# Experts' x tiles from the fifth on, transposed by a transfer of two-byte planes

## The chip, the core and the metric

One core of one Trainium2 chip runs the kernel. The metric is the device time of one execution in microseconds (us); lower is better.

## The reference

Three stages follow one another; all data are float32.

```python
x = _attn_ref(q, k, v, mem_k, mem_v)     # windowed attention, 4 x 8 x 768 x 64, as rows: 3072 x 512
x = _moe_ref(x, w_in, w_out, a, b)       # h = x @ w_in (2048); rational function of h; @ w_out (512)
# last stage, 8 experts of 1024:
logits = x @ w_gate
expert_idx = argmax(logits, 1)
for e in range(8):
    xe = x[expert_idx == e]
    out[expert_idx == e] = gate_w[:, None] * (maximum(xe @ w1[e], 0) @ w2[e])
```

## The kernel before, in words

Every float32 product is made in three parts: an operand is split into an upper part (rounded by ScalarE) and a lower part (the rest, by VectorE), and upper x upper, upper x lower and lower x upper are summed in PSUM. The stages before the experts end at about 670 us. They leave the rows of x sorted by expert in DRAM (`rows_by_expert`, 514 columns: 512 of x, the gate weight and the row's number), in tiles of 128 rows. The run has 27 tiles of 5 experts, the largest expert first.

The expert stage runs one loop on each engine (`Fori(2, ...)`), which share counters only through semaphores; each engine's work is in the order in which it is written. Tiles 0 to 3 are written out ahead of the loop. Body t of TensorE's loop (lines 816 to 829) is: `transpose_h(t)`, 8 transposes of the hidden layer into PSUM; `first_product(t + 1)`, 24 matmuls with 512 columns, x of the next tile by w1; `transpose_x(t + 2)` (line 535), 4 transposes of the gathered rows into PSUM; `second_product(t)`, 24 matmuls, h by w2.

ScalarE in body t (1035 to 1042): `upper_h(t)`, the upper part of the transposed h; where the schedule says so, `split_expert`, upper parts of 8 chunks of the next expert's weights (128x1024 each; `x_raw` is chunk 0, `e_raw` the seven others); `relu(t + 1)`; `upper_x(t + 2)` in two halves. VectorE (1411 to 1417): `lower_h(t)`, the lower parts of the same 8 chunks, `lower_x(t + 2)`, and `finish(t)`, which multiplies y by the gate weight. `first_product(t + 2)` of the next body waits for `xg_lo_done`, that is for `lower_x(t + 2)`, half by half. The weights' reloads are issued by SyncE as chunks come free (line 507).

POOL (1565 to 1570) in body t: `fetch(t + 3)`, which keeps two columns of the rows before, waits until TensorE has transposed them (`tx_done`) and issues the load of the next 128 rows into `xg`; `land_y(t - 1)` waits for the last store; `copy_idx(t)`; `send_y(t)` waits for `finish(t)` and issues the scatter of y.

Of the kernel before, what the change touches and what calls it, by code (L numbers as in the profile page):

```python
# [15 lines left out]
F32, F32R, BF16, I32, U32 = (mybir.dt.float32, mybir.dt.float32r, mybir.dt.bfloat16,  # L16
                             mybir.dt.int32, mybir.dt.uint32)
ALU = mybir.AluOpType
# [6 lines left out]
P = 128  # L25
# [166 lines left out]
def build(nc, qk_all, v_all, w_mlp, w_exp, w_gate, coef, consts, sights, out):  # L192
# [4 lines left out]
    with ExitStack() as ctx:  # L197
# [80 lines left out]
        with ExitStack() as ph:  # L278
            xg_hi = sb("xg_hi", [P, KT, P], F32R, ph)
            xg_lo = sb("xg_lo", [P, KT, P], F32R, ph)  # L280
# [15 lines left out]
        with ExitStack() as ph:  # L296
            sb("below_ge", [P, 2 * KT * P + (WCH - 1) * CW + 3 * EF + DM], F32, ph)
            ge = sb("ge", [P, 3, TMAX, E], F32, ph)
# [44 lines left out]
        meta_copied, gathered, tx_done = (sem(n) for n in ("meta_copied", "gathered", "tx_done"))  # L343
        xg_hi_done, xg_lo_done, w1e_done = sem("xg_hi_done"), sem("xg_lo_done"), sem("w1e_done")
# [166 lines left out]
        def _(pe):  # L511
# [304 lines left out]
            with pe.Fori(2, before_last) as t:  # L816
# [6 lines left out]
                transpose_x(t + 2)  # L823
# [11 lines left out]
            pe.sem_inc(tx_done, 2)  # L835
# [20 lines left out]
        def _(act):  # L856
# [68 lines left out]
            def upper_x(t):  # L925
# [4 lines left out]
                for c in range(2):  # L930
                    act.wait_ge(tx_done, t * 2 + (c + 1))
                    act.activation(xg_hi[:, 2 * c:2 * c + 2].rearrange("p k t -> p (k t)"),  # L932
                                   PS[:, x_halves(t)[c], 2 * c * P:2 * (c + 1) * P], ACT.Copy).then_inc(xg_hi_done, 1)

# [100 lines left out]
            with act.Fori(2, last_tile) as t:  # L1035
                act.wait_ge(w2e_done, upto(w2e_done, t))
                upper_h(t)
                nxt = load_sched(act, R_SPLIT, t, 0, E - 1)
# [3 lines left out]
                upper_x(t + 2)  # L1042
# [5 lines left out]
        def _(dve):  # L1048
# [108 lines left out]
            def lower_x(t):  # L1157
# [5 lines left out]
                for c in range(2):  # L1163
                    dve.wait_ge(xg_hi_done, t * 2 + (c + 1))
                    dve.tensor_tensor(xg_lo[:, 2 * c:2 * c + 2].rearrange("p k t -> p (k t)"),  # L1165
                                      PS[:, x_halves(t)[c], 2 * c * P:2 * (c + 1) * P],
                                      xg_hi[:, 2 * c:2 * c + 2].rearrange("p k t -> p (k t)").bitcast(F32),
# [243 lines left out]
            with dve.Fori(2, last_tile) as t:  # L1411
# [4 lines left out]
                lower_x(t + 2)  # L1416
# [6 lines left out]
        def _(pool):  # L1423
# [30 lines left out]
            def keep_meta(t):  # L1454

                pool.wait_ge(gathered, t * 16 + 16)
                pool.tensor_copy(meta_of(t, slice(0, 2)), xg[:, DM:XW]).then_inc(meta_copied, 1)

# [102 lines left out]
            tiles = load_sched(pool, R_CNT, 0, NSUB, TILES)  # L1561
            fetch(4, col)
            send_y(1)
            fetched, before_last, last_tile = tiles_less(pool, 3), tiles_less(pool, 2), tiles_less(pool, 1)
            with pool.Fori(2, fetched) as t:
                fetch(t + 3, col_of(t + 3))
                land_y(t - 1)
                copy_idx(t)
                pool.drain()
# [3 lines left out]
            pool.wait_ge(gathered, tiles * 16)  # L1573
            pool.tensor_copy(meta_of(last_tile, slice(0, 2)), xg[:, DM:XW]).then_inc(meta_copied, 1)
# [86 lines left out]
```

## Time and profile before

| | us |
|---|---|
| median of 3 runs | 997.41 (997.26 to 997.83) |
| profiled execution, own time | 995.93 |
| its span, first to last instruction | 993.9 |
| TensorE busy | 976.4 (98%) |
| VectorE busy | 619.0 (62%) |
| ScalarE busy | 580.9 (58%) |
| POOL busy | 403.9 (41%) |
| mean granted TensorE clock | 0.999 of full |

The times of rows below count from the span's start. PE is TensorE's matmuls and PEld its weight loads, DVE is VectorE, ACT ScalarE, SP SyncE; a q behind the name (ACTq) is the engine's instruction queue, where issues of transfers and scalar operations are. L541 is line 541. Busy time of an engine says nothing by itself of what waits for what; the chain of waits does: it goes back from the last instruction, at each step to what released it.

### The profile page before, as it was taken

To read this page: it belongs to the slowest core of one execution; us is meant where nothing else is said; L and a number is where in the kernel's file an instruction comes from. 1 tells how busy PE (TensorE), PEld (TensorE's weight loads), DVE (VectorE), ACT (ScalarE), POOL (GpSimd) and SP (SyncE) were. 2 spreads that over 40 slices of the span, in tenths; PEclk is the share of its full clock that TensorE was granted. 3 is DMA by queue.
4 is the path that set the end of the run, shared out by engine and by line. 5 is a ranking of instruction groups with operands and counts; after the bars stand their busy time and mean duration, and the time that the engine had idled before them with its cause. 6 is when DMAs were issued, how large, how long until landed. Compare 5 with 4: busy or idle time off the path is not lost. (4 is left out here: it accounts for less than half of the span.)

```text
span 993.9 us, 19287 instructions
## 1 busy us (share of the span) xinstructions
PE 976.4 (98%) x6102; PEld 797.9 (80%) x6103; DVE 619.0 (62%) x1073; ACT 580.9 (58%) x1248; POOL 403.9 (41%) x393
## 2 busy tenths in 40 slices
PE   7999999999999999999999999999999999999997
PEld 5787778888887888888888888887888888888886
DVE  6786788767876876697678778862524324325222
ACT  6998787766676676676676767831524224225221
POOL 2886454444654464446446544732111111111111
PEclk9999999999999999999999999999999999999999
DMA  8999415920990194059001301215812412411100
GB/s 288 392 398 402 175 43 180 367 91 1 306 362 10 59 369 166 0 173 335 0 0 42 116 24 40 67 43 165 281 47 78 176 42 75 169 42 42 33 32 26
DMA packets 58031, 140.49 MB, mean 141 GB/s; under 512 B 4663, under 2 KB 10423, under 8 KB 57984
## 3 DMA queue, kind: packets, MB, share of 16 engines
q1 hardware_dynamic: 51120, 119.06, 33.8%
q0 software_dynamic: 6560, 20.77, 6.2%
q8 instruction: 28, 0.46, 0.2%
q14 instruction: 19, 0.16, 0.0%
q10 hardware_dynamic: 304, 0.04, 0.0%
HBM read 68.32 MB, written 72.32 MB: 142 GB/s over the span
## 5 line engine op out<-in xcount | busy, mean ns | idle before, releaser
L524 PE MATMUL PS<-xs,weights 128*128 (+1 forms) x1152 | 280.8, 392 | 0.0
L524 PEld LDWEIGHTS PS<-xs,weights 128*128 128x128 f32 x1152 | 213.6, 188 | 44.0
L686 PE MATMUL PS<-weights,g_hi 128*128 128x512 f32 x768 | 237.9, 391 | 0.9 <-POOL g_lo L1497 0.3
L1497 POOL TENSOR_TENSOR g_lo<-g_sb,g_hi 128x512 fp32r<-128x512 f32 x96 | 125.1, 1303 | 263.7 <-ACT g_hi L993 263.7
L686 PEld LDWEIGHTS PS<-weights,g_hi 128*128 128x128 f32 x768 | 143.0, 188 | 34.3 <-POOL g_lo L1497 2.8
L686 PE MATMUL PS<-weights,g_lo 128*128 128x512 f32 x384 | 149.5, 389 | 0.0
L974 ACT ACTIVATE b_ln<-PS,cf 128x512 f32<-128x512 f32 x96 | 66.0, 687 | 131.2 <-PE PS L524 131.2
L567 PE MATMUL PS<-weights,h_hi 128*128 (+1 forms) x432 | 136.2, 396 | 1.4 <-DVE h_lo L1174 1.4
L558 PE MATMUL PS<-weights,xg_hi 128*128 (+1 forms) x432 | 136.2, 396 | 0.8 <-issue 0.5
L1500 POOL TENSOR_TENSOR den<-den,b_r 128x512 f32<-128x512 f32 x96 | 128.1, 1334 | 3.9 <-ACT b_r L1001 3.6
L1210 DVE SCALAR_TENSOR_TENSOR den<-den,b_r 128x512 f32<-128x512 f32 x96 | 66.0, 687 | 76.6 <-POOL den L1500 76.5
L567 PEld LDWEIGHTS PS<-weights,h_hi 128*128 128x128 f32 x432 | 79.0, 188 | 17.4 <-issue 1.4
L558 PEld LDWEIGHTS PS<-weights,xg_hi 128*128 128x128 f32 x432 | 79.0, 188 | 17.0 <-issue 1.2
L1165 DVE TENSOR_TENSOR xg_lo<-PS,xg_hi 128x256 fp32r<-128x256 f32 x52 | 19.6, 418 | 116.5 <-ACT xg_hi L932 116.5
L944 ACT ACTIVATE h_sb<-PS 128x1024 f32<-128x1024 f32 x27 | 27.6, 1023 | 110.2 <-PE PS L558 110.2
L939 ACT ACTIVATE h_hi<-PS 128x512 fp32r<-128x512 f32 x54 | 29.3, 596 | 104.3 <-PE PS L551 104.3
L1531 POOL DMA_INDIRECT out<-y_sb,idx_s x27 | 27.5, 1018 | 149.3 <-DVE y_sb L1186 146.3
L558 PE MATMUL PS<-weights,xg_lo 128*128 (+1 forms) x216 | 84.6, 392 | 0.0
L567 PE MATMUL PS<-weights,h_lo 128*128 (+1 forms) x216 | 84.5, 391 | 0.0
L686 PEld LDWEIGHTS PS<-weights,g_lo 128*128 128x128 f32 x384 | 72.1, 188 | 15.2
L980 ACT ACTIVATE num<-PS,neg_a 128x512 f32<-128x512 f32 x96 | 74.9, 780 | 0.0
L1246 DVE SCALAR_TENSOR_TENSOR den<-b_ln,b_r 128x512 f32<-128x512 f32 x96 | 66.0, 688 | 13.8 <-ACT b_r L977 11.6
(209 smaller groups left out, 1511.2 us busy)
## 6 DMA issues: line engine op xcount, KB each, us to landing
rows_by_expert<-pad_rows SPq DMA_DIRECT2D x16, 1799.0 KB
e_raw<-w_exp SPq DMA_DIRECT2D x34, 512.0 KB, 6.5
qk<-qk_all SPq DMA_DIRECT2D x32, 420.0 KB, 6.1
rows_by_expert<-pad_rows SPq DMA_DIRECT2D x8, 1542.0 KB
vw<-v_all SPq DMA_DIRECT2D x32, 384.0 KB, 6.2
rows_by_expert<-pad_rows SPq DMA_DIRECT2D x8, 1285.0 KB
w_raw<-w_mlp SPq DMA_DIRECT2D x16, 512.0 KB, 7.6
pad_rows<-rows_by_expert POOLq DMA_DIRECT2D x27, 257.0 KB
```

Of the source, the lines that this page charges most:

```text
L524: last = pe.matmul(PS[:, H_BANK + f % 2, :], w[:, wp], rhs, start=k == 0, stop=k == 3 * KT - 1)
L558: last = pe.matmul(PS[:, half, :], xp[:, kt, :], w_half(off, kt, wp, half), start=n == 0, stop=n == 3 * KT - 1, skip_group_check=True)
L567: last = pe.matmul(PS[:, y_bank(t), :], hp[:, ft, :], w_half(off, KT + ft // 2, wp, ft % 2), start=ft == 0 and k == 0, stop=ft == EKT - 1 ...
L686: last = pe.matmul(PS[:, ACC_BANK + s, :], gp[:, f % 2, s * P:(s + 1) * P], w[:, wp], start=f == 0 and k == 0, stop=f == FT - 1 and k == 2)
L939: act.activation(hi[:, 4 * c:4 * c + 4].rearrange("p k t -> p (k t)"), PS[:, h_banks(t)[c], :], ACT.Copy).then_inc(h_hi_done, 1)
L944: act.activation(h_sb[:], PS[:, 0:2, :].rearrange("p a n -> p (a n)"), ACT.Relu).then_inc(relu_done, 1)
L974: act.activation(b1_ln[:], PS[:, hb, :], ACT.Abs, scale=cf[:, 4:5]).then_inc(b12_done, 1)
L980: act.activation(num[:, par], PS[:, hb, :], ACT.Identity, scale=neg_a[:, 3:4], bias=neg_a[:, 2:3]).then_inc(u_done, 1)
L1210: dve.scalar_tensor_tensor(den[:, q], den[:, q], -2.0, b2_r0[:, q], ALU.add, ALU.mult).then_inc(w_done, 1)
L1246: dve.scalar_tensor_tensor(den[:, par], b1_ln[:], 1.0 + 1e-6, b2_r0[:, par], ALU.add, ALU.add).then_inc(q_ready, 1)
L1497: pool.tensor_tensor(g_lo[:, q], g_sb[:], g_hi[:, q].bitcast(F32), ALU.subtract).then_inc(g_lo_done, 1)
L1500: pool.tensor_tensor(den[:, st.m % 2], den[:, st.m % 2], b2_r0[:, st.m % 2], ALU.mult).then_inc(t_ready, 1)
```

## The change

For tiles 4 and up TensorE no longer transposes x. POOL parts the gathered rows (each float32 is two 16-bit halves) into two planes, all lower halves and all upper halves (`planes`, 1,024 two-byte elements a partition; `part_x`). ScalarE's queue issues one transfer that transposes the 8 blocks of 128 x 128 two-byte elements from `planes` to `mirrored` within SBUF (`turn_x`), behind `upper_h` and ahead of `split_expert`. VectorE joins the halves again to float32 in `xt`, in two copies, behind its splits (`join_x`); then `upper_turned` and `lower_turned` make `xg_hi` and `xg_lo` from `xt` in SBUF, as `upper_x` and `lower_x` did from PSUM. `xt` lies where `xg_lo` lies, so the join also waits until the product of the tile before is over (`w1e_done`). The load of the next rows waits for POOL's own parting (`load_next`) in place of TensorE's transposes. ScalarE's and VectorE's loops run one turn past the last tile, so POOL raises `planes_done` once more.

```diff
@@ -277,6 +277,8 @@
             count = sb("count", [P, E], F32, ph)
         with ExitStack() as ph:
             xg_hi = sb("xg_hi", [P, KT, P], F32R, ph)
+            with ExitStack() as over:
+                xt = sb("xt", [P, KT, P], F32, over)
             xg_lo = sb("xg_lo", [P, KT, P], F32R, ph)
             e_raw = sb("e_raw", [P, WCH - 1, CW], F32, ph)
             h_hi = sb("h_hi", [P, EKT, P], F32R, ph)
@@ -295,6 +297,9 @@
             h1_lo = sb("h1_lo", [P, EKT, P], F32R, ph)
         with ExitStack() as ph:
             sb("below_ge", [P, 2 * KT * P + (WCH - 1) * CW + 3 * EF + DM], F32, ph)
+            with ExitStack() as over:
+                planes = sb("planes", [P, 2 * DM], U16, over)
+                mirrored = sb("mirrored", [P, 2 * KT, P], U16, over)
             ge = sb("ge", [P, 3, TMAX, E], F32, ph)
             gt = sb("gt", [P, E, SLOTS], F32, ph)
             per = sb("per", [P, 8, E], F32, ph)
@@ -341,6 +346,7 @@
         e_hi_done, e_lo_done = sem("e_hi_done"), sem("e_lo_done", WCH)
         led.append((e_lo_done, WCH))
         meta_copied, gathered, tx_done = (sem(n) for n in ("meta_copied", "gathered", "tx_done"))
+        planes_done, planes_turned, xt_done, turn_go = (sem(n) for n in ("planes_done", "planes_turned", "xt_done", "turn_go"))
         xg_hi_done, xg_lo_done, w1e_done = sem("xg_hi_done"), sem("xg_lo_done"), sem("w1e_done")
         relu_done, th_done, h_hi_done, h_lo_done = sem("relu_done"), sem("th_done"), sem("h_hi_done"), sem("h_lo_done", 1)
         w2e_done, gate_copied, y_done = sem("w2e_done", 1), sem("gate_copied"), sem("y_done", 1)
@@ -820,7 +826,6 @@
                 transpose_h(t)
                 first_product(t + 1)
                 order, off = load_sched(pe, R_ORD, t, 1, E), load_sched(pe, R_OFF, t, 0, WCH)
-                transpose_x(t + 2)
 
                 pe.wait_ge(h_lo_done, upto(h_lo_done, t * 2 + 2))
                 pe.wait_ge(y_done, upto(y_done, t))
@@ -832,7 +837,6 @@
             pe.wait_ge(h_lo_done, upto(h_lo_done, t * 2))
             transpose_h(t)
             first_product(last_tile)
-            pe.sem_inc(tx_done, 2)
             order, off = load_sched(pe, R_ORD, t, 1, E), load_sched(pe, R_OFF, t, 0, WCH)
             pe.wait_ge(h_lo_done, upto(h_lo_done, t * 2 + 2))
             pe.wait_ge(y_done, upto(y_done, t))
@@ -931,6 +935,18 @@
                     act.wait_ge(tx_done, t * 2 + (c + 1))
                     act.activation(xg_hi[:, 2 * c:2 * c + 2].rearrange("p k t -> p (k t)"),
                                    PS[:, x_halves(t)[c], 2 * c * P:2 * (c + 1) * P], ACT.Copy).then_inc(xg_hi_done, 1)
+
+            def turn_x(t):
+
+                act.wait_ge(planes_done, t - (FIRST_TILES - 1))
+                act.sem_inc(turn_go, 1)
+                act.dma_start(mirrored[:], planes[:], transpose=True).then_inc(planes_turned, 16)
+
+            def upper_turned(t):
+                for c in range(2):
+                    act.wait_ge(xt_done, (t - FIRST_TILES) * 2 + (c + 1))
+                    act.activation(xg_hi[:, 2 * c:2 * c + 2].rearrange("p k t -> p (k t)"),
+                                   xt[:, 2 * c:2 * c + 2].rearrange("p k t -> p (k t)"), ACT.Copy).then_inc(xg_hi_done, 1)
 
             def upper_h(t):
                 hi = h_tiles(t)[0]
@@ -1035,11 +1051,12 @@
             with act.Fori(2, last_tile) as t:
                 act.wait_ge(w2e_done, upto(w2e_done, t))
                 upper_h(t)
+                turn_x(t + 2)
                 nxt = load_sched(act, R_SPLIT, t, 0, E - 1)
                 with act.If(nxt > 0):
                     split_expert(nxt)
                 relu(t + 1)
-                upper_x(t + 2)
+                upper_turned(t + 2)
             act.wait_ge(w2e_done, upto(w2e_done, last_tile))
             upper_h(last_tile)
 
@@ -1167,6 +1184,22 @@
                                       xg_hi[:, 2 * c:2 * c + 2].rearrange("p k t -> p (k t)").bitcast(F32),
                                       ALU.subtract).then_inc(xg_lo_done, 1)
 
+            def join_x(t):
+
+                dve.wait_ge(planes_turned, (t - (FIRST_TILES - 1)) * 16)
+                dve.wait_ge(w1e_done, t)
+                for c in range(2):
+                    dve.tensor_copy(xt[:, 2 * c:2 * c + 2].bitcast(U16).rearrange("p k (t w) -> p k t w", w=2),
+                                    mirrored[:].rearrange("p (w k) t -> p k t w", w=2)[:, 2 * c:2 * c + 2]).then_inc(xt_done, 1)
+
+            def lower_turned(t):
+                for c in range(2):
+                    dve.wait_ge(xg_hi_done, t * 2 + (c + 1))
+                    dve.tensor_tensor(xg_lo[:, 2 * c:2 * c + 2].rearrange("p k t -> p (k t)"),
+                                      xt[:, 2 * c:2 * c + 2].rearrange("p k t -> p (k t)"),
+                                      xg_hi[:, 2 * c:2 * c + 2].rearrange("p k t -> p (k t)").bitcast(F32),
+                                      ALU.subtract).then_inc(xg_lo_done, 1)
+
             def lower_h(t):
                 hi, lo = h_tiles(t)
                 for c in range(2):
@@ -1413,7 +1446,8 @@
                 nxt = load_sched(dve, R_SPLIT, t, 0, E - 1)
                 with dve.If(nxt > 0):
                     split_expert(nxt)
-                lower_x(t + 2)
+                join_x(t + 2)
+                lower_turned(t + 2)
                 finish(t)
             lower_h(last_tile)
             finish(last_tile, last_y)
@@ -1455,6 +1489,20 @@
 
                 pool.wait_ge(gathered, t * 16 + 16)
                 pool.tensor_copy(meta_of(t, slice(0, 2)), xg[:, DM:XW]).then_inc(meta_copied, 1)
+
+            def part_x(t):
+
+                keep_meta(t)
+                if not isinstance(t, int):
+                    pool.wait_ge(planes_turned, (t - FIRST_TILES) * 16)
+                    pool.sem_inc(rows_go, 1)
+                pool.tensor_copy(planes[:].rearrange("p (w n) -> p n w", w=2),
+                                 xg[:, 0:DM].bitcast(U16).rearrange("p (n w) -> p n w", w=2)).then_inc(planes_done, 1)
+
+            def load_next(t, col):
+
+                pool.wait_ge(planes_done, t - FIRST_TILES)
+                pool.dma_start(xg[:, 0:XW], tiles_dram[bass.ds(col, 1)].rearrange("o p n -> (o p) n")).then_inc(gathered, 16)
 
             def load_tile(t, col):
 
@@ -1558,20 +1606,20 @@
             copy_idx(1)
             pool.wait_ge(sched_ready, 1)
             col = col_of(4)
-            tiles = load_sched(pool, R_CNT, 0, NSUB, TILES)
             fetch(4, col)
+            part_x(4)
             send_y(1)
             fetched, before_last, last_tile = tiles_less(pool, 3), tiles_less(pool, 2), tiles_less(pool, 1)
             with pool.Fori(2, fetched) as t:
-                fetch(t + 3, col_of(t + 3))
+                load_next(t + 3, col_of(t + 3))
                 land_y(t - 1)
                 copy_idx(t)
+                part_x(t + 3)
                 pool.drain()
                 send_y(t)
             land_y(fetched - 1)
             finish_y(fetched)
-            pool.wait_ge(gathered, tiles * 16)
-            pool.tensor_copy(meta_of(last_tile, slice(0, 2)), xg[:, DM:XW]).then_inc(meta_copied, 1)
+            pool.sem_inc(planes_done, 1)
             finish_y(before_last)
             finish_y(last_tile, True)
```

## Rows read from the trace of the kernel before

**Rows 1.** The page, parts 1 and 2: TensorE's busy time and share; granted clock by slice.

```profile
PE 976.4 (98%) x6102; PEld 797.9 (80%) x6103; DVE 619.0 (62%) x1073; ACT 580.9 (58%) x1248; POOL 403.9 (41%) x393
...
PEclk9999999999999999999999999999999999999999
```

**Rows 2.** Chain of waits, an ordinary expert body: start us, length us, engine, output, line.

```profile
853.62 5.49 PE PS L567 x24
859.12 0.87 PE PS L551 x8
...
865.48 0.44 PE PS L541 x4
```

**Rows 3.** Groups of instructions, 690 to 990: busy us, mean ns, idle before.

```profile
L1291 DVE TENSOR_TENSOR weights<-e_raw,weights 128x1024 f32 x28 | 32.1, 1217 | 0.0
```

**Rows 4.** Timeline, a body with splits: start us, us, engine, line, operation [idle before].

```profile
761.05 1.09 ACT L939 ACTIVATE h_hi<-PS 128x512 fp32r<-128x512 f32 x2 [4.79 <-PE PS L551]
...
763.84 1.23 DVE L1291 TENSOR_TENSOR weights<-x_raw,weights 128x1024 f32 x1 [0.87 <-ACT weights L923]
764.98 8.03 DVE L1291 TENSOR_TENSOR weights<-e_raw,weights 128x1024 f32 x7
772.93 0.74 DVE L1165 TENSOR_TENSOR xg_lo<-PS,xg_hi 128x256 fp32r<-128x256 f32 x2
...
768.63 1.02 POOL L1520 CAST idx_s<-meta 128x1 uint32 x1
```

**Rows 5.** Chain of waits, the same body.

```profile
760.57 0.87 PE PS L551 x8
...
773.74 2.39 PE PS L558 x10
```

**Rows 6.** Chain of waits, end of the first body with splits.

```profile
711.73 0.30 issue
```

**Rows 7.** Timeline, an ordinary body, VectorE and POOL.

```profile
854.56 0.76 DVE L1165 TENSOR_TENSOR xg_lo<-PS,xg_hi 128x256 fp32r<-128x256 f32 x2 [4.94 <-ACT xg_hi L932]
...
854.88 0.20 POOL L1520 CAST idx_s<-meta 128x1 uint32 x1
860.77 1.02 POOL L1531 DMA_INDIRECT out<-y_sb,idx_s  x1 [5.69 <-DVE y_sb L1186]
```

**Rows 8.** Single lines that issue transfers: duration of the issue ns min/median/max, starts.

```profile
L859 ACTq DMA_DIRECT2D sight<-sights x2: 261/419/577, 0.9 to 1.5; - x2
...
L507 SPq DMA_DIRECT2D e_raw<-w_exp x21: 332/333/756, 706.6 to 847.0; - x21
...
L476 SPq DMA_DIRECT2D rows_by_expert<-pad_rows x32: 507/3514/8428, 160.0 to 450.7; - x32
```

**Rows 9.** Landing: weights (line 507); stores of y (the view of DMA issues).

```profile
DMA to landing us min/median/max: 3.3/6.7/10.9
...
out<-y_sb,idx_s POOLq DMA_INDIRECT x27, 2.8
```

**Rows 10.** Lines with a one-source VectorE operation; groups by form.

```profile
L1056 DVE CAST mask<-sight x2: 441/443/445, 4.6 to 5.2; 4x576 bf16<-4x576 f32 x2
...
L1204 DVE COPY x<-PS 128x512 f32<-128x512 f32 x10 | 6.4, 682 | 0.1
```

**Rows 11.** Groups by form, POOL.

```profile
L1446 POOL CAST weights<-w_raw 128x1024 fp32r<-128x1024 f32 x5 | 5.2, 1038 | 0.0
```

**Rows 12.** Timeline, POOL ahead of the expert loop.

```profile
684.92 0.59 POOL L1464 DMA_DIRECT2D pad_rows<-rows_by_expert  x1 [3.17 <-PE PS L541]
687.94 1.03 POOL L1531 DMA_INDIRECT out<-y_sb,idx_s  x1 [2.43 <-issue]
```

**Rows 13.** Line 1154, the first expert's splits: duration ns min/median/max.

```profile
L1154 DVE TENSOR_TENSOR weights<-e_raw,weights x6: 1217/1394/2312, 603.7 to 653.1; 128x1024 fp32r<-128x1024 f32 x6
```

**Rows 14.** Window of an ordinary body: busy us by engine, clock, DMA share, GB/s.

```profile
852.00:864.00 12.00, 12.00 (x61) 9.98 (x60) 2.85 (x6) 2.67 (x5) 1.98 (x4) 1.00 0.26 96
```

**Rows 15.** Waits of TensorE from 690 on: us in total, times, longest us.

```profile
PE PS L567 <- DVE h_lo L1174: 1.2, 1, 1.2
```

More of the change, by code:

```diff
@@ L14 @@
 import concourse.mybir as mybir
-F32, F32R, BF16, I32, U32 = (mybir.dt.float32, mybir.dt.float32r, mybir.dt.bfloat16,
-                             mybir.dt.int32, mybir.dt.uint32)
+F32, F32R, BF16, I32, U32, U16 = (mybir.dt.float32, mybir.dt.float32r, mybir.dt.bfloat16,
+                                  mybir.dt.int32, mybir.dt.uint32, mybir.dt.uint16)
 ALU = mybir.AluOpType
```

## Prediction

> **What bounds the kernel now.** The page first: TensorE is busy in 98% of the span and its granted clock is at full speed in all 40 slices [rows 1], so what counts is what TensorE does and when it is kept waiting. The chain of waits over an ordinary expert body is TensorE alone [rows 2]: transpose h (0.87 us), first product (24 matmuls of the same kind as the second, 5.49), transpose x (0.44), second product (5.49), together 12.29 us. There are 23 such bodies (t = 2 to 24), and each holds one transpose of x, so the removed instructions lie on the path: 4 x about 0.11 us issued, 0.44 us, and no engine covers them.
>
> Four of the 23 bodies also split an expert's weights (28 splits from e_raw in the loop, seven to a body [rows 3], and one each from x_raw ahead of them). Read one on each engine [rows 4], with T the start of its transposes of h, 760.57 [rows 5]: ScalarE ends upper_h at T+1.6 and goes on to the splits; VectorE waits 0.87 us for the first, starts at 763.84, works without a gap and ends at 773.01 (T+12.4); then it makes xg_lo, the first half done at 773.34. TensorE begins the product that needs it at 773.74 [rows 5]. So the spare time of VectorE in such a body is about 0.4 us, some 0.3 after the hand-off; in the first of the four there is none, TensorE idles 0.30 there [rows 6]. Ordinary bodies have 5 us of idle time ahead of xg_lo [rows 7].
>
> **Removed.** 23 x 0.44 = 10.1 us of TensorE if nothing is late next. In the 19 ordinary bodies I take it whole: 19 x 0.44 = 8.4 us. In the four others TensorE would only arrive 0.44 us earlier at a product whose operand isn't there.
>
> **Added, in an ordinary body.** ScalarE issues the transfer behind upper_h, T+1.6. Its price there, d, is not shown by any transposing transfer. Rows around it: this engine's own small loads took 0.26 to 0.58 us to issue, SyncE's of 512 KB 0.33, and the clearing transfers, 896 runs or more each, 0.51 to 8.4 us with a median of 3.5 (their queue full) [rows 8]. The new one moves 256 KB as 8 blocks for 128 partitions, at least 1,024 runs. The row nearest in runs is the clearing one; between its minimum and its median I take d = 2.0, with ends 0.4 and 3.5. The Trainium skill ("DMA: Bandwidth & Descriptors", in "Why a DMA increments its semaphore by 16 and not by 1") speaks against the change here: a transposing transfer within SBUF costs the older sequencers 262,144 cycles for 8,192 tiles, 32 a tile, beside 512 for a plain transfer and 631 for a small transposing one. The trace shows 0.33 us for a plain one, so 0.65 ns a cycle; were a tile 16 rows by 128 elements, as that page's "DMA Transpose (X-bar)" suggests, there would be 64 tiles, 631 + 2,048 cycles, an estimate of 1.7 us, and the sum would be 2 us to the slow side. No row here shows a transposing one.
>
> From the end of the issue to landing I take 3 us (the store of y lands in 2.8 at the median, 512 KB of weights in 6.7, at most 10.9 [rows 9]). So the planes are there at T+6.6. VectorE may join them from T+6.4 on (first product over, w1e_done). Two joins of 512 two-byte elements: a cast of 576 elements within SBUF took 443 ns, a copy of 512 from PSUM 682 [rows 10]; ends 0.8 and 1.4 together, I take J = 0.83 (SBUF to SBUF, as the first row). With upper_turned beside the second join and half of lower_turned (0.4) behind, xg_lo's first half is done 1.4 us after the join starts, T+8; the product needs it at T+11.85+0.87 = T+12.7. The transfer has room to T+11.3, that is X = 9.7 us from issue to landing. relu on ScalarE comes at T+6.4 and is not behind an issue of 2 to 3.5 us. So an ordinary body pays nothing.
>
> POOL: load_next no longer waits for TensorE's transposes, it is issued behind the store of y, at T+2.7 [rows 7], and the rows land about T+6.4 (3 us as the store, and its own 0.6); part_x waits for the transfer before (T+6.6); 1,024 two-byte elements cost 1.04 us at the rate of its cast [rows 11], 2.1 if two-byte writes go at half of it. Behind it waits send_y, whose y comes only at T+12.7; idle time ahead of it was 5.7 us [rows 7]. Hidden. In front of the loop part_x(4) stands before send_y(1): the rows asked for at 684.92 are there at 688 and parted at 689.5, so y of tile 1 leaves about 2 us later than at 687.94 [rows 12]; its next user is finish(2), at the end of the second product of t = 2 (711.73 less 0.87 and a body of 12.29: 698.6 [rows 2, 6]). Tile 4's planes are turned near 694.5, needed joined at about 699. Hidden, with 2 us left. The 24th turn, of a tile that doesn't exist, is released by POOL about T+4.5 of the last body and joined ahead of finish, which isn't due before T+11.85: nothing.
>
> **Added, in a splitting body.** All of it is in VectorE's full queue. (1) ScalarE's first split starts d later; VectorE already waits for that split, so its whole chain ends d later: 2.0. (2) The joins stand behind the splits and ahead of xg_lo: 0.83. (3) part_x meets the splits: an earlier split of the same size took 1.39 us at the median and 2.31 at most beside POOL's work, 1.22 at least, and POOL's cast of one column took 1.02 instead of 0.20 among the splits [rows 4, 7, 13]. Ends 0 and 1.1, I take 0.3, since POOL's copy is about as long as one split. Less the spare 0.3: 2.83 us added per body (the 0.44 gained is already used up in arriving early), three times, and 3.13 in the first: 11.6. What follows (finish, lower_h) has over 3 us until its product.
>
> **Sum.** -8.4 + 11.6 = +3.2 us. The profiled execution's span of 993.9 becomes 997.1, its own time 995.93 becomes 999.1. The median of the runs lies 1.5 us above that execution; on it I forecast 1000.6 us. Less than 0.2%, 2 us, can't be told from no change.
>
> **Rivals.**
> Cheap issue (other side): the ACT queue issues the transfer as fast as its others, d = 0.44. Its place is the four splitting bodies; each then costs 0.83 + 0.44 + 0.3 - 0.3 = 1.3, 5.4 with the first, against 8.4 gained: 994.4. It decides from d under 0.7 (then over 2 us are gained). For: the only rows of ACT's queue. Against: they move 128 runs or fewer. Chance 0.29. Between d = 0.7 and 1.7 the two sums cancel within 2 us: 0.17, time about 997.
>
> The transfer itself lands too late: above X = 9.7 every body stalls by the excess, since the join stands between landing and product. At the longest landing of the rows, 10.9 [rows 9], each ordinary body pays 1.2 - 0.44: 19 x 0.76 = 14.4, and with the 11.6 of the splitting bodies, whose joins come later than any landing, it is 1023. Against: that landing had seven transfers of 512 KB in flight; DMA engines are 26% busy in an ordinary stretch [rows 14]. Chance 0.10. The Trainium skill ("VectorE: DVE Perf Modes", "The three transpose paths") gives 1309 ns for 128x128 two-byte elements by DMA against 390 on TensorE, and advises TensorE where PSUM will do. Eight blocks one after another would be an estimate of 10.5 us, which is this rival at about 1016.
>
> TensorE's clock: the stalls of some 3.3 us (2.83 + 0.44) are longer than any idle time of the expert stretch; 1.2 us of it left the granted clock where it was [rows 1, 15]. If it fell to the lower level (1.2 of 2.4 GHz) for one product, 5.49 would be 11, four times: +22, 1023. Chance 0.03. The Trainium skill ("TensorE: Matmul & The Clock Gate", "Why this matters for your kernels") warns of gaps between bursts for this reason; no run here shows such a fall.
>
> The forecast itself, d of 1.7 to 3.5: 0.41. That the transposes stay on TensorE is excluded: only tiles up to 3 keep them.
>
> **Range.** Best of the bounds: d 0.44, J 0.8, no contention: 8.4 - 4 x 0.94 - 0.3 = 4.3 gained, 993.1. Worst without rivals: 3.5 + 1.4 + 1.1 - 0.3 = 5.7 per body, 23.1 less 8.4, 1012. I take 992.5 to 1018, half way into the late transfer. Faster 0.29, same 0.17, slower 0.41 + 0.10 + 0.03 = 0.54.
>
> **What would show it.** (a) Ordinary bodies of 11.85 us without a gap in TensorE: right; a wait for xg_lo there: the transfer is late. (b) ScalarE's issue behind upper_h: 2 us, and the first split of the four bodies later by it. (c) Joins of 0.4 us each. (d) TensorE idle about 3.3 us ahead of the product after each splitting body. Under 1.7 us of it, the kernel is faster and my d is wrong. (e) The same clock throughout. (f) part_x of 1 to 2.6 us, and y never late for TensorE.

## The result, and the profile after

The changed kernel takes 1030.91 us (median of 3 runs, 1029.08 to 1030.97) against 997.41: ratio 1.0327, 95% interval 1.0302 to 1.0352. It is slower by 33 us where 3 were forecast, outside the range. The profiled execution took 1029.08 us, span 1027.2.

The page, parts 1 and 2 (compare [rows 1]):

```profile
PE 977.3 (95%) x6010; PEld 796.6 (78%) x6011; DVE 720.1 (70%) x1121; ACT 584.0 (57%) x1248; POOL 521.4 (51%) x416
...
PEclk9999999999999999999999999998998999898999
```

TensorE has some 90 instructions fewer and is busy 0.9 us longer, and four slices late in the span no longer show full speed. VectorE is busy 101 us more, POOL 118. The groups of instructions by form, 690 to 1000, say where:

```profile
L1499 POOL COPY planes<-pad_rows 128x1024 uint16<-128x1024 uint16 x23 | 116.2, 5053 | 0.1
L1198 DVE TENSOR_TENSOR xg_lo<-xt,xg_hi 128x256 fp32r<-128x256 f32 x46 | 64.6, 1440 | 9.3 <-ACT xg_hi L948 8.7
L1324 DVE TENSOR_TENSOR weights<-e_raw,weights 128x1024 f32 x28 | 44.2, 1646 | 0.0
L1192 DVE COPY xt<-mirrored 128x512 uint16<-128x512 uint16 x46 | 41.8, 951 | 88.5 <-PE PS L564 76.5 <-DMA mirrored<-planes 12.0
```

POOL's parting takes 5 us each time, and three kinds of VectorE work have grown in the mean: the splits from 1,217 ns [rows 3] to 1,646, beside xg_lo and the joins. A mean hides the shape of it. Line 1324 in one splitting body, then line 1499 over the whole span (duration min/median/max), and the timeline of that body:

```profile
L1324 DVE TENSOR_TENSOR weights<-e_raw,weights x7: 1209/1210/5244, 779.7 to 790.6; 128x1024 f32 x7
```

```profile
L1499 POOL COPY planes<-pad_rows x23: 4692/4880/5887, 689.6 to 986.4; 128x1024 uint16<-128x1024 uint16 x23
```

```profile
769.12 4.85 POOL L1499 COPY planes<-pad_rows 128x1024 uint16<-128x1024 uint16 x1
...
769.34 4.61 DVE L1198 TENSOR_TENSOR xg_lo<-xt,xg_hi 128x256 fp32r<-128x256 f32 x2 [0.60 <-ACT xg_hi L948]
...
774.45 1.27 ACTq L943 DMA_TRANSPOSE mirrored<-planes  x1
...
778.56 1.22 DVE L1324 TENSOR_TENSOR weights<-x_raw,weights 128x1024 f32 x1 [2.52 <-ACT weights L927]
...
779.71 12.05 DVE L1324 TENSOR_TENSOR weights<-e_raw,weights 128x1024 f32 x7
...
780.92 5.88 POOL L1499 COPY planes<-pad_rows 128x1024 uint16<-128x1024 uint16 x1
...
791.69 0.75 DVE L1192 COPY xt<-mirrored 128x512 uint16<-128x512 uint16 x2
...
792.58 0.76 DVE L1198 TENSOR_TENSOR xg_lo<-xt,xg_hi 128x256 fp32r<-128x256 f32 x2
...
793.25 1.21 PE L564 MATMUL PS<-weights,xg_hi 128*128 x2 [6.27 <-DVE xg_lo L1198]
```

Six of the seven splits take the old 1.21 us and one takes 5.24: it isn't slowed down, it is held, by 4.03, beside the parting of 780.92 to 786.80. Two halves of xg_lo, 0.84 us of work, are held for 4.61 in the ordinary body ahead (769.34) and end with the parting of 769.12, at 773.97. In an ordinary body that costs nothing, there were 4.94 us of idle time [rows 7]. In a splitting one everything is behind it, and TensorE stands for 6.27 us.

What TensorE does after that, in windows (busy us and count of PE, PEld, DVE, ACT, POOL, then granted clock, DMA share, GB/s):

```profile
788.00:793.00 5.00, 0.00 (x0) 0.00 (x0) 4.85 (x8) 0.87 (x3) 0.00 (x0) 0.75 0.88 258
793.00:797.00 4.00, 3.75 (x9) 2.98 (x10) 2.36 (x6) 0.97 (x2) 1.11 (x2) 0.50 0.98 361
797.00:801.00 4.00, 4.00 (x19) 3.26 (x18) 0.07 (x1) 0.07 (x1) 1.66 (x4) 0.95 0.59 169
```

The granted clock is 0.50 (1.2 GHz) for the first 4 us of the product, which does 9 matmuls there instead of 19. The chain of waits has that product and the next:

```profile
793.25 7.64 PE PS L564 x24
...
807.22 5.45 PE PS L564 x24
```

7.64 us for the same 24 matmuls: 2.15 lost after the stall of 6.3. The products behind the other two later splitting bodies take 8.50 and 8.08 us. And TensorE waits in a second place, ahead of its transposes of h behind the splits; the waits have it (total, times, longest):

```profile
PE PS L557 <- ACT h_sb L960: 2.2, 3, 0.7
```

ScalarE writes `h_sb` (relu) behind its own splits, which start later because of the issue.

**Where the 33.3 us of span went**, from the starts of the transposes of h. An ordinary body lasts 11.78 us (12.29 before): some 15 of them, -7.6. The prelude is 0.9 longer. The first splitting body and the one behind it took 38.97 us, 25.13 before: +13.8. The three later pairs took 32.96, 33.80 and 33.39 instead of 24.7: +26.1.

### The profile page after: what moved, and what is told of

The parts are those of the page before. It is cut to its first block and busy times, and to the rows that moved or that the text cites. A ratio compares the mean times of both kernels' runs of the same rounds, so it can differ in the third digit from the quotient of the medians.

```text
span 1027.2 us, 19309 instructions
## 1 busy us (share of the span) xinstructions
PE 977.3 (95%) x6010; PEld 796.6 (78%) x6011; DVE 720.1 (70%) x1121; ACT 584.0 (57%) x1248; POOL 521.4 (51%) x416
## 3 DMA queue, kind: packets, MB, share of 16 engines
q1 hardware_dynamic: 51120, 119.06, 33.3%
## 5 line engine op out<-in xcount | busy, mean ns | idle before, releaser
L564 PE MATMUL PS<-weights,xg_hi 128*128 (+1 forms) x432 | 144.6, 417 | 29.9 <-DVE xg_lo L1198 29.4
L573 PE MATMUL PS<-weights,h_hi 128*128 (+1 forms) x432 | 133.5, 390 | 1.4 <-DVE h_lo L1207 1.4
L564 PEld LDWEIGHTS PS<-weights,xg_hi 128*128 128x128 f32 x432 | 84.6, 202 | 48.6 <-issue 31.3
L1499 POOL COPY planes<-pad_rows 128x1024 uint16<-128x1024 uint16 x23 | 116.2, 5053 | 0.1
L1192 DVE COPY xt<-mirrored 128x512 uint16<-128x512 uint16 x48 | 42.6, 929 | 94.1 <-PE PS L564 76.5
L564 PE MATMUL PS<-weights,xg_lo 128*128 (+1 forms) x216 | 88.5, 409 | 0.0
L1279 DVE SCALAR_TENSOR_TENSOR den<-b_ln,b_r 128x512 f32<-128x512 f32 x96 | 66.0, 688 | 13.8 <-ACT b_r L993 11.6
L1248 DVE SCALAR_TENSOR_TENSOR g_sb<-num,neg_a,den 128x512 f32<-128x512 f32 x96 | 72.2, 752 | 3.8
```

The source lines that it names most:

```text
L564: last = pe.matmul(PS[:, half, :], xp[:, kt, :], w_half(off, kt, wp, half), start=n == 0, stop=n == 3 * KT - 1, skip_group_check=True)
L573: last = pe.matmul(PS[:, y_bank(t), :], hp[:, ft, :], w_half(off, KT + ft // 2, wp, ft % 2), start=ft == 0 and k == 0, stop=ft == EKT - 1 ...
L1248: dve.scalar_tensor_tensor(g_sb[:], num[:, q], neg_a[:, 0:1], den[:, q], ALU.add, ALU.mult).then_inc(g_ready, 1)
L1279: dve.scalar_tensor_tensor(den[:, par], b1_ln[:], 1.0 + 1e-6, b2_r0[:, par], ALU.add, ALU.add).then_inc(q_ready, 1)
L1499: pool.tensor_copy(planes[:].rearrange("p (w n) -> p n w", w=2), xg[:, 0:DM].bitcast(U16).rearrange("p (n w) -> p n w", w=2)).then_inc(pla ...
```

## The experiments

Runs of one line of reasoning stand together. Times are medians; each ratio is against runs of the kernel before on the same chip.

**1. Take the parting away.** From tile 5 on POOL copies 2 elements instead of 1,024, so the data of these tiles are left out; all else stays.

```diff
-                pool.tensor_copy(planes[:].rearrange("p (w n) -> p n w", w=2), ...).then_inc(planes_done, 1)
+                if isinstance(t, int):
+                    pool.tensor_copy(planes[:].rearrange("p (w n) -> p n w", w=2), ...).then_inc(planes_done, 1)
+                else:
+                    pool.tensor_copy(planes[:, 0:2], xg[:, 0:1].bitcast(U16)).then_inc(planes_done, 1)
```

> Left out: POOL parts only two of the 1,024 elements from tile 5 on; waits, transfer, joins and the rest are as in the changed kernel. Theory A (POOL's 4.9 us copy holds up VectorE's operations that read two SBUF operands or run in its faster one-source mode, until the copy ends): the eight splits are back at 9.2 us in a row, joins 0.8 us, TensorE idles about 2.6 us after each splitting body (later first split 1.65, joins 0.83, 0.44 of its own, less 0.3), its clock stays full; 997.4 - 19 x 0.51 + 4 x 2.2 + 0.3 = about 997. Theory B (the transposing transfer and its joins are what is late, the copy only looks long): little changes, 1023 to 1030.

Measured: 1008.51 us, ratio 1.0111 (1.0079 to 1.0143). The groups of VectorE:

```profile
L1324 DVE TENSOR_TENSOR weights<-e_raw,weights 128x1024 f32 x28 | 32.1, 1219 | 0.0
L1192 DVE COPY xt<-mirrored 128x512 uint16<-128x512 uint16 x48 | 18.4, 425 | 92.4 <-PE PS L564 74.8 <-DMA mirrored<-planes 17.6
L1198 DVE TENSOR_TENSOR xg_lo<-xt,xg_hi 128x256 fp32r<-128x256 f32 x48 | 18.3, 423 | 11.6 <-ACT xg_hi L948 10.7
```

All three are back at their own length, so the parting, which shares no data with the splits, was what held them; it is 22 of the 33 us. But 1008.5 is not the 997 expected. The windows behind the stall (2.25 us here) say why:

```profile
780.00:782.00 2.00, 0.32 (x1) 0.32 (x2) 1.76 (x7) 1.44 (x4) 0.00 (x0) 1.00 1.03 416
782.00:784.00 2.00, 2.00 (x6) 1.60 (x5) 1.87 (x3) 0.40 (x1) 0.45 (x1) 0.52 1.04 424
```

The clock falls here as well; a product takes 7.36 us (chain of waits) instead of 5.49. The later pairs last 12.67 + 15.98 = 28.65 us. Without the 1.87 of clock they are 2.1 above the 24.7 of before: what the prediction's terms give without contention, 2.0 + 0.83 - 0.3 - 0.44 = 2.1 for a pair.

**2. The same parting in eight instructions** of 64 columns, as long in sum.

```diff
+                for k in range(8):
+                    last = pool.tensor_copy(whole[:, 64 * k:64 * k + 64], xg[:, 64 * k:64 * k + 64]...)
+                last.then_inc(planes_done, 1)
```

> The same parting as eight POOL instructions of 64 columns. Theory A1 (VectorE waits for the one POOL instruction that runs): no split, join or subtraction is held for more than about 0.6 us at a time, the longest is under 2 us, and the total falls to 1000 to 1012. Theory A2 (VectorE gets nothing as long as POOL has work of this kind in a row): some operations still take 4 us or more, 1028 to 1032.

Measured: 1020.90 us, ratio 1.0217 (1.0183 to 1.0252). The time lies between the two theories; the holds are those of A1, no split of the body below took over 1.31 us. Timeline of a splitting body:

```profile
778.10 8.50 DVE L1324 TENSOR_TENSOR weights<-e_raw,weights 128x1024 f32 x7
...
779.31 9.67 POOL L1501 COPY planes<-pad_rows 128x128 uint16<-128x128 uint16 x8
...
786.53 1.85 DVE L1192 COPY xt<-mirrored 128x512 uint16<-128x512 uint16 x2
```

The splits lose 0.47 us instead of 4.02: the hold lasts as long as the one POOL instruction that is running, and no piece stands before more than one split. POOL pays in turn, as it did in the body above (5.88 us for a parting of 4.88): 1.2 us a piece (9.67 by 8), where in an ordinary body (767.44) the eight took 4.87 together, 0.61 each: it waits for VectorE's instructions too. The joins (0.76 before, here 1.85) are held by the last pieces, TensorE still idles up to 3.7 us, and the clock still falls.

**3. The parting alone, in the kernel before.** TensorE goes on transposing; POOL makes the same copy, which nothing reads, ahead of the load of the next rows.

```diff
             with pool.Fori(2, fetched) as t:
-                fetch(t + 3, col_of(t + 3))
+                keep_meta(t + 2)
+                pool.tensor_copy(planes[:].rearrange("p (w n) -> p n w", w=2), ...).then_inc(planes_done, 1)
+                pool.wait_ge(planes_done, t - 1)
+                load_tile(t + 3, col_of(t + 3))
```

> The kernel before with one thing added: POOL's parting copy of the gathered rows (its result isn't read), ahead of the load of the next rows; tiles are still transposed by TensorE. Theory A: one of the eight splits in each splitting body is held for about 4 us, TensorE idles about 4 us behind each, 4 x 3.7 = 15, and 8 more if the clock falls there: 1012 to 1021. Theory B: hidden, 997 to 999.

Measured: 1021.19 us, ratio 1.0215 (1.0184 to 1.0247). Timeline of a splitting body:

```profile
773.46 4.99 POOL L1571 COPY planes<-pad_rows 128x1024 uint16<-128x1024 uint16 x1
...
773.93 4.92 DVE L1295 TENSOR_TENSOR weights<-x_raw,weights 128x1024 f32 x1 [0.87 <-ACT weights L927]
```

The copy alone, without any transfer, join or missing transpose, costs 23 us. A split that takes 1.23 [rows 4] ends at 778.85, just behind the copy's end, 778.45. xg_lo here reads one operand from PSUM. Only one pair of its halves fell beside a copy:

```profile
693.49 4.86 POOL L1571 COPY planes<-pad_rows 128x1024 uint16<-128x1024 uint16 x1
...
697.73 0.76 DVE L1169 TENSOR_TENSOR xg_lo<-PS,xg_hi 128x256 fp32r<-128x256 f32 x2 [5.92 <-ACT xg_hi L936]
```

It started while the copy had 0.6 us to run, and took its usual 0.76. In run 2 h_lo, which also reads PSUM, took its usual 1.29 us at 749.31 with pieces running until 749.77. So, over these runs, VectorE's operations with both operands in SBUF were held, and in the changed kernel its copies within SBUF too (joins of up to 5.1 us); those with one operand in PSUM weren't, in the few places where they met the copy.

The Trainium skill ("SBUF — State Buffer", "Who interferes with whom") says of VectorE's two-port copies against POOL: "Whoever issues first gets the shared pair for the whole instruction; the other **fully blocks** (not throttle)." It says there too that an operation with two SBUF inputs contends with a POOL instruction that reads SBUF, and one with at most one SBUF input, outside the two-port modes, doesn't. Runs 2 and 3 agree, in both directions (5.88 for 4.88 us on POOL, 4.92 for 1.23 on VectorE) and on the exception (0.76 us). The prediction didn't use it.

**4. The transfer alone, in the kernel before.** ScalarE issues the transposing transfer at its place; nobody reads it.

```diff
                 upper_h(t)
+                act.wait_ge(planes_turned, t * 16)
+                act.sem_inc(turn_go, 1)
+                act.dma_start(mirrored[:], planes[:], transpose=True).then_inc(planes_turned, 16)
```

> The kernel before with one thing added: the transposing transfer, issued by ScalarE behind upper_h in every body (constant planes, the result isn't read). Theory A: the first split of the four splitting bodies starts 1.65 us later, 4 x 1.65 less 0.9 of spare time: +5.7, 1003, no idle time elsewhere. Theory B (the transfer disturbs others: POOL's gathers, the weights' loads, VectorE): beyond 1010.

Measured: 1005.22 us, ratio 1.0065 (1.0042 to 1.0087). Timeline, and the windows around the product's start:

```profile
764.21 1.27 ACTq L1044 DMA_TRANSPOSE mirrored<-planes  x1
...
768.30 1.22 DVE L1299 TENSOR_TENSOR weights<-x_raw,weights 128x1024 f32 x1 [2.77 <-ACT weights L927]
...
778.10 0.73 PE L562 MATMUL PS<-weights,xg_hi 128*128 x2 [1.37 <-DVE xg_lo L1173]
```

```profile
776.00:778.00 2.00, 0.72 (x7) 0.48 (x5) 2.00 (x4) 1.13 (x3) 0.00 (x0) 1.00 0.97 377
778.00:780.00 2.00, 1.90 (x8) 1.62 (x9) 1.91 (x5) 0.00 (x0) 0.10 (x1) 1.00 1.01 408
```

The issue takes 1.27 us, and VectorE waits 1.9 us longer for the first split than before (0.87, [rows 4]); TensorE then stands for 1.4. That stall leaves the granted clock at 1.00; the one of 2.25 in run 1 was followed by 0.52, and by a product 1.9 us longer. A splitting body with the next lasts 12.67 + 13.99 = 26.66 us here, 2.0 above before.

**5. The clock alone.** In the changed kernel TensorE gets 90 small matmuls, whose result nobody reads, ahead of the product that waits.

```diff
                 transpose_h(t)
+                after_split = load_sched(pe, R_SPLIT, t - 1, 0, E - 1)
+                with pe.If(after_split > 0):
+                    for _ in range(90):
+                        pe.matmul(PS[:, 7, 0:P], ones[:], tri[:], start=True, stop=True, ...)
                 first_product(t + 1)
```

> The changed kernel with 90 matmuls of 128 columns (their result isn't read) on TensorE in the body behind each splitting one, ahead of the waiting product, about 5 of the 6.4 us that it idles there. Theory A (the fall of the granted clock after the idle time is its own cost): the product behind the wait takes 5.5 us instead of 7.3 to 8.5, about 9 us in all: 1021. Rival (that product is slow for another reason, the weights' loads or its operands): unchanged, 1029 to 1031.

Measured: 1021.77 us, ratio 1.0247 (1.0228 to 1.0267). A window behind the stall:

```profile
794.00:798.00 4.00, 4.00 (x19) 3.31 (x19) 1.92 (x3) 0.44 (x1) 1.58 (x2) 1.00 1.07 303
```

19 matmuls in 4 us at 1.00, where the changed kernel did 9. The three later pairs shrink from 33.4 to 31.05 us each, 7 in all; the medians differ by 9.1, the profiled executions by 6.5. The first pair gains 0.6 only: its first product still takes 7.97, 2.5 over its 5.49, and ahead of the second the added matmuls themselves end late. There the changed kernel's products took 8.2 and 7.3, some 4 us more than 5.49 each. So of the 33 us some 11 are the clock: 7 given back here, and 4 read from the lengths of those two.

**6. The parting on ScalarE.** It has no part in the holds seen so far. It parts behind relu; tile 4 is parted by VectorE.

```diff
                 relu(t + 1)
+                part_x(t + 3)      # act.activation(planes "p (w n) -> p n w", xg "p (n w) -> p n w", ACT.Copy)
                 upper_turned(t + 2)
```

> The changed kernel with the parting on ScalarE, behind relu (tile 4's on VectorE ahead of the loop) instead of on POOL; all tiles are computed in full. Theory A (POOL's copy held VectorE; what is left is the issue on ScalarE and the joins): no VectorE operation is held, the splits take 9.2 us in a row, TensorE idles 2.5 us ahead of the product behind each splitting body and the clock still falls there, as without parting: a pair of bodies 28.7 us instead of 24.7; 998 - 15 x 0.51 + 4 x 4 = 1006. Rival (parting costs wherever it is done, through the chain parting, transfer, joining): 1015 or more.

Measured: 1034.16 us, ratio 1.0375 (1.0358 to 1.0391). The groups:

```profile
L944 ACT ACTIVATE planes<-pad_rows 128x1024 uint16<-128x1024 uint16 x22 | 106.5, 4839 | 2.7 <-POOL meta L1503 2.6
L1333 DVE TENSOR_TENSOR weights<-e_raw,weights 128x1024 f32 x28 | 32.1, 1217 | 0.0
L1454 DVE COPY planes<-pad_rows 128x1024 uint16<-128x1024 uint16 x1 | 2.9, 2949 | 2.2 <-POOL meta L1503 2.2
```

No split is held any more (1,217 ns). But the copy takes 4.84 us on ScalarE too, xg_hi stands behind it, and TensorE now waits in ordinary bodies: 22 waits instead of 5. So POOL isn't slow at this copy; the copy is slow. Its writes alternate between two places 1 KB apart.

A variant of it with the transfer issued by SyncE, so that ScalarE is free of the issue (`turn_x` moved to SyncE's loop, which now goes over tiles):

> As the run before, and the transposing transfer is issued by SyncE's queue, whose loop over experts becomes one over tiles (reloads of weights stand behind the transfer of the same body). Theory A: ScalarE's first split is at its old place, of the additions only the joins (0.83 us, less 0.3 spare) are left in VectorE's full queue; TensorE idles about 1.1 us behind each splitting body, too little for the clock to fall; 998 - 7.7 + 4 x 0.0 = about 990, faster than the kernel before. Rival (the transfer lands late behind the weights' loads in the same queue): waits for it in the body after a splitting one, 995 to 1000.

Measured: 1023.43 us, ratio 1.0264 (1.0247 to 1.0282). Missed for the same reason: 4,866 ns a parting, ordinary bodies of 12.5 us. The issue took 1.24 us there, 1.27 on ScalarE. Its three later splitting bodies also show that a long stall isn't always followed by a low clock: behind stalls of 2.73 and 2.71 us the products took 7.2 us, behind one of 2.77 (TensorE starts again at 931.41) 5.6, in this window:

```profile
932.00:936.00 4.00, 4.00 (x19) 3.33 (x18) 1.60 (x3) 0.00 (x0) 1.59 (x2) 1.00 0.50 129
```

**7. The same bytes in another order.** The changed kernel with POOL's copy walked plane by plane; each write is then beside the last and each read steps by 4 bytes.

```diff
-                pool.tensor_copy(planes[:].rearrange("p (w n) -> p n w", w=2),
-                                 xg[:, 0:DM].bitcast(U16).rearrange("p (n w) -> p n w", w=2)).then_inc(planes_done, 1)
+                pool.tensor_copy(planes[:].rearrange("p (w n) -> p w n", w=2),
+                                 xg[:, 0:DM].bitcast(U16).rearrange("p (n w) -> p w n", w=2)).then_inc(planes_done, 1)
```

> The changed kernel with POOL's parting copy walked in another order: one plane after the other, so that each plane is written from end to end and the source is read in steps of 4 bytes, in place of writes that alternate between two places 1 KB apart. Same instruction count and elements. Theory C (the 4.8 us, the same on POOL and on ScalarE, come from the alternating two-byte writes): the copy takes 1.0 to 1.5 us, VectorE is held at most that long, and the total is near that of the run without parting: 1008 to 1011. Theory D (two-byte elements cost 4.7 ns each on POOL in any order): 4.8 us again and 1029 to 1031.

Measured: 1008.76 us, ratio 1.0107 (1.0081 to 1.0133): 22 us from an order of two letters.

```profile
L1499 POOL COPY planes<-pad_rows 128x1024 uint16<-128x1024 uint16 x23 | 30.4, 1320 | 0.1
L1324 DVE TENSOR_TENSOR weights<-e_raw,weights 128x1024 f32 x28 | 35.5, 1335 | 0.0
```

The time is that of run 1, which had no copy; the splits are still held, by 0.12 us each in the mean. Two things changed with the order: the writes no longer alternate, and the copy no longer goes in runs of two elements. The join parts them in part, on VectorE: it too goes in runs of two, its reads alternate between places 1 KB apart and its writes run straight, and it takes 0.42 us for 512 elements (run 1), 0.8 ns each. VectorE's own parting took 2.9 ns each (2,949 for 1,024, run 6), and 0.7 plane by plane (694, run 8c). So there the runs of two aren't what costs, and the alternating writes are; on POOL and ScalarE no run separates the two. The Trainium skill speaks of this as well ("SBUF — State Buffer", "Door 1: The DMA port swizzle"): SBUF has lines of 16 bytes, and each access that goes to another line pays. For writes the order agrees, 4.88 against 1.32 us; the join's alternating reads, 0.8 ns an element, show no such price.

**8. Both cures together**, to find a version that beats the kernel before. In all three the copy has the new order.

```diff
  (a) ScalarE parts behind relu, SyncE issues the transfer
  (b) POOL parts, SyncE issues the transfer
  (c) ScalarE parts behind relu and issues the transfer behind upper_turned, for the tile after:
                 relu(t + 1)
+                part_x(t + 3)
                 upper_turned(t + 2)
+                turn_x(t + 3)
```

(a) 

> Parting on ScalarE in that other order, the transfer issued by SyncE. Theory C: the copy takes about 1.05 us on ScalarE, xg_hi is no longer late in ordinary bodies (they are 11.8 us), and of the additions only the joins are left in VectorE's full queue: TensorE idles about 1.1 us behind a splitting body, too little for the clock to fall: about 990. Theory D: as the run with ScalarE's parting in the old order, 1023.

(b) 

> As the changed kernel, parting on POOL in the other order and the transfer issued by SyncE. Theory C: as the run before plus one hold of VectorE of up to 1 us in each splitting body; idle time of about 2.1 us there, where the clock may fall or not: 991 without, 998 with. Theory D: 1020 or more.

(c) 

> Parting on ScalarE plane by plane, and the transposing transfer again on ScalarE's queue, but of the next tile and behind upper_turned, at the end of a body, where ScalarE has nothing to do; so it is neither ahead of the splits nor behind the weights' loads in SyncE's queue. Theory A (what SyncE's version still lost was one transfer of tile 6 that landed after 10.9 us behind 4 MB of weights, 4 us; the rest of its bodies stay): ordinary bodies 11.8 us, a splitting one 13.3, the body after the first splitting one about 12 to 13 instead of 15.7: 992 to 993, faster than the kernel before by 5. Rival (the issue at the end of a splitting body delays upper_h of the next and with it the second product): 996 to 999.

Measured: (a) 996.26 us, ratio 0.9988 (0.9971 to 1.0004); (b) 1001.28, 1.0028 (1.0011 to 1.0046); (c) 995.53, 0.9976 (0.9961 to 0.9992). Only (c) is faster than the kernel before, by 0.24%, at the edge of what can be told. In (a) the transfer of an early tile stood among SyncE's loads of weights; the chain of waits has it:

```profile
715.19 10.91 DMA mirrored<-planes
```

In (b) POOL's copy still meets VectorE (joins of 709 ns instead of 425) and the clock still falls behind stalls of up to 2.8 us. Of (c), groups, the wait of TensorE (total, times, longest), and the chain:

```profile
L943 ACT ACTIVATE planes<-pad_rows 128x1024 uint16<-128x1024 uint16 x24 | 25.1, 1046 | 7.1 <-POOL meta L1510 7.1
L1340 DVE TENSOR_TENSOR weights<-e_raw,weights 128x1024 f32 x28 | 32.1, 1219 | 0.0
```

```profile
PE PS L564 <- DVE xg_lo L1214: 5.8, 4, 2.0
```

```profile
716.06 7.31 PE PS L564 x24
```

The splits are whole, the issue is out of their way, and the four waits are 5.8 us in sum (29.4 after). A later splitting body with the next lasts 11.8 + 13.3 = 25.1, 0.4 above before: TensorE stands for 1.3 us (the joins and its own earlier arrival, less the spare), and the two removed transposes give 1.0 back. The first splitting body and the next take 27.96 us against 25.13, with a clock fall behind 2.02 us of idle time in it, and the loop starts 2.7 us later (688.1 against 685.4), for which I have no experiment; over the runs here it starts between 685.4 and 689.0.

**9. The next rows earlier.** (c) with POOL issuing the load of the next rows ahead of the store of y, against the late parting in the first bodies.

```diff
                 part_x(t + 3)
+                load_next(t + 4, col_of(t + 4))
                 pool.drain()
                 send_y(t)
```

> As the run before (parting on ScalarE plane by plane, the next tile's transfer issued behind upper_turned), and POOL issues the load of the next rows as soon as the rows before are parted, ahead of send_y instead of behind it. Theory: what is left is one late chain in front (rows of tile 5 were asked for only behind the store of tile 1 and its register work, parted 3 us later than they could be, so the transfer stood ahead of the splits of the first splitting body: 2.0 us of idle time, and 1.9 of lower clock). It comes 1.5 to 2 us earlier: the body after the first splitting one takes 12 to 13.5 us instead of 15.7, all others as before: 991 to 994, ratio 0.994 to 0.996. Rival (ScalarE's upper_h of that body is bound by something else): unchanged, ratio 0.998.

Measured: 1001.53 us, ratio 1.0035 (1.0017 to 1.0052): missed, on the other side. Timeline of the second body with a late product:

```profile
716.28 0.19 POOL L1584 CAST idx_s<-meta 128x1 uint32 x1 [6.20 <-DMA out<-y_sb,idx_s]
...
716.81 1.06 ACT L943 ACTIVATE planes<-pad_rows 128x1024 uint16<-128x1024 uint16 x1 [4.66 <-POOL meta L1511]
...
718.87 1.21 PE L564 MATMUL PS<-weights,xg_hi 128*128 x2 [5.50 <-DVE xg_lo L1214]
```

The rows were there, but the store of y now lands late, and POOL, in its order, waits for it before it copies the meta data that releases ScalarE's parting; xg_hi stands behind that parting. One wait was traded for a longer one.

## Why the prediction was wrong

The direction was right, and so was the place, the splitting bodies, with VectorE's full queue as the main cause. Within it one mechanism was wrong (POOL's copy doesn't slow VectorE, it holds it), one was left out of the sum (the clock), and one early chain was timed too short (tile 4). The forecast missed by 30 us: the three later pairs cost 6.3 us more each than its terms (hold 4.0 instead of 0.3, clock 2.6 instead of nothing), the first pair 11 more.

**The term that failed: contention in a splitting body, "part_x meets the splits ... Ends 0 and 1.1, I take 0.3".** It measured 4.0 (one split of 5,244 ns). Two steps led there. The copy was sized by the rate of a cast, 1.04 to 2.1 us [rows 11]; it took 4.88, because of the order in which it was walked (run 7: 1.32 for the same bytes). And its effect was read from slowed medians, 1.39 us [rows 13], as if the engines shared a rate; it is a hold to the end of the other's instruction (runs 2, 3). The rows had the sign of it: the maximum of 2.31 in [rows 13], and POOL's cast of one column, 1.02 instead of 0.20 [rows 4, 7], about as long as the rest of a split. Run 1 gives back 4.8 us in each later pair (4.0 of hold, and 0.8 because its shorter stalls cost less clock, products of 7.3 instead of 8.1) and 9.3 in the first (38.97 less 29.7), and starts its loop 1.6 later: 22. A later pair's 8.7 us are then 2.1 of forecast terms, 4.0 of hold and 2.6 of clock (the products of 7.64, 8.50 and 8.08, less 5.49).

**The clock, a rival at 0.03.** The forecast itself had stalls of 3.3 us, and 2.02 to 2.25 were enough (runs 1, 8), though not every time: 1.91 in run 8b and 2.77 in run 6's variant left the clock at 1.00. As a term it is 1.8 to 3.0 us a stall, some 11 in all in five falls, not the 22 of that rival: the granted clock is back at 1.00 some 4 to 6 us into the product, which loses 2 to 3 us, not 5.5. The one stall of the kernel before, 1.2 us [rows 15], was taken for more than it showed.

**"Hidden, with 2 us left", tile 4.** It wasn't. POOL parts it from 689.63 to 694.49, as against 1 us; the issue is at 694.61; the planes land 6.3 us later, among the loads of weights, and the join starts at 701.05, where it was due at about 699. Then xg_lo is held for 4.5 by the parting of tile 5. The timeline of after:

```profile
689.63 4.86 POOL L1499 COPY planes<-pad_rows 128x1024 uint16<-128x1024 uint16 x1
...
701.05 0.76 DVE L1192 COPY xt<-mirrored 128x512 uint16<-128x512 uint16 x2 [12.00 <-DMA mirrored<-planes]
...
701.79 4.69 POOL L1499 COPY planes<-pad_rows 128x1024 uint16<-128x1024 uint16 x1
701.96 4.52 DVE L1198 TENSOR_TENSOR xg_lo<-xt,xg_hi 128x256 fp32r<-128x256 f32 x2
```

What held:
- (a) Ordinary bodies: 11.78 us without a gap, 11.85 forecast; all of the removed time is gained, 0.51 each.
- (b) The issue sits behind upper_h and takes 1.27 us, and it delays the first split by 1.9 (run 4), 2.0 forecast. That this fits so well is in part luck: 2.0 was taken between 0.4 and 3.5 from transfers of another kind, and the issue alone would have been 1.27. By the cycles of the Trainium skill ("DMA: Bandwidth & Descriptors", "Why a DMA increments its semaphore by 16 and not by 1") it was an estimate of 1.7, above the 1.27 measured; the rival of a cheap issue, under 0.7, falls.
- (c) Joins: 0.42 us each when not held (run 1).
- (d) TensorE idles 2.25 us ahead of the product where nothing is held (3.3 forecast), 6.3 with the hold. Another 0.7 it idles ahead of its transposes, for ScalarE's relu; the forecast had put everything in VectorE's queue.
- Landing: 3.1 us at the median (3 forecast), so the rival of a late transfer falls for ordinary bodies, and so does the price of eight blocks one after another, 10.5. One early tile did land as late when the transfer sat in SyncE's queue (10.91), among loads of weights.
- (f) failed in its first half: the parting took 4.9 us, not 1 to 2.6.

## What to carry to other kernels

Before a copy is put on POOL, look for what VectorE does beside it with two operands in SBUF, or from SBUF to SBUF: each such operation can lose the whole length of the POOL instruction, so price the hold by the longest single instruction, and add it where VectorE is full. Price a copy by the order of its writes too, not by its count of elements alone, and let the write side run straight. And when a forecast has TensorE idle for 2 us or more ahead of a product, add the clock to the sum: 2 to 3 us a stall here, in most cases.

## What the runs showed of the hardware

- Parting 1,024 two-byte elements a partition, writes alternating between places 1 KB apart: 4.88 us on POOL, 4.84 on ScalarE, 2.95 on VectorE. Plane by plane: 1.32 (1.25 in run 8b), 1.05 and 0.69.
- A VectorE operation with both operands in SBUF and a POOL copy within SBUF hold each other for the length of the instruction: 1.2 us became 4.92 and 5.24; eight POOL pieces of 0.61 took 1.2 each. With one operand in PSUM, 0.76 and 1.29 us as without the copy.
- TensorE idle for 1.4 and 1.9 us: granted clock 1.00 after it. For 2.02 and 2.25 us: 0.5, from within the first 2 us behind it. For 2.77 us, once: 1.00.
- A transposing transfer of 256 KB within SBUF: 1.27 us to issue from ScalarE (whose next work started 1.9 later than without it), 1.24 from SyncE at the median, landed after 3.1 at the median and 6.3 to 10.9 among loads of weights.
